# Normalising two chunks ahead in a spare scratch, a reordered end of the tile on ScalarE, and the products dealt over four steps

## The reference

```
mag = sqrt(a_re^2 + a_im^2); scale = min(mag, 0.999) / (mag + 1e-6)
a_re, a_im = a_re * scale, a_im * scale                  # "normalising"
for t in range(768):
    S = (a_re + i a_im)[t] * S + outer(k[t], v[t])        # complex state per head
    y[t] = q[t] @ real(S)
h = y @ w_in; e = exp(h - max(h)); solu = h * e / sum(e)
x = layernorm(solu) * g_ln @ w_out
noisy = x @ w_gate + softplus(x @ w_noise) * noise; top 2 experts, their softmax weights
out = sum over the token's 2 experts of weight * relu(x @ w1[e]) @ w2[e]
```

## Time and profile before

| | us |
|---|---|
| three runs | 1211.77, 1214.07, 1214.28 |
| median | 1214.07 |
| the profiled execution, its own time | 1212.83 |
| its span from first to last instruction | 1211.1 |
| PE busy, share of the span | 1041.4 (86%) |
| DVE busy | 872.8 (72%) |
| ACT busy | 621.1 (51%) |
| POOL busy | 449.7 (37%) |

### The profile page before, as it was taken

The page is one execution under the profiler, slowest core; times in us unless marked ns, Lnnn a source line. Parts: engine busy times, 40 slices in busy tenths (PEclk is TensorE's granted clock), DMA queues, the critical chain, the costliest instruction groups (busy, mean ns, idle before and its releaser), DMA issues.

```text
span 1211.1 us, 21883 instructions
## 1 busy us (share of the span) xinstructions
PE 1041.4 (86%) x7866; PEld 984.5 (81%) x7866; DVE 872.8 (72%) x1729; ACT 621.1 (51%) x967; POOL 449.7 (37%) x417
## 2 busy tenths in 40 slices
PE   0046988988998998899964999999999999999996
PEld 0035887877887887788864999999999999999996
DVE  6888779879969969945553777667676767776672
ACT  6432663764664664544532555555555555555551
POOL 4110241252352352243523244345434533543442
PEclk9977998998898898899986999999999999999998
DMA  9420220230230210211404666767676767676640
GB/s 231 174 76 27 54 86 27 67 86 27 66 87 27 64 37 27 58 42 53 125 14 156 227 233 226 253 234 256 202 267 235 253 227 244 228 230 235 209 162 1
DMA packets 85980, 167.51 MB, mean 138 GB/s; under 512 B 18566, under 2 KB 57696, under 8 KB 85872
## 3 DMA queue, kind: packets, MB, share of 16 engines
q1 hardware_dynamic: 72432, 137.71, 36.1%
q0 software_dynamic: 13440, 28.40, 6.4%
HBM read 148.83 MB, written 21.92 MB: 141 GB/s over the span
## 4 chain that ended last, share of the span: by engine, by line
PE 55%; issue 2%; ACT 1%; DVE 1%; DMA 1%; POOL 0%; POOLq 0%; DVEq 0%; ACTq 0%; SPq 0%
PE bank L1367 22%; PE bank L1547 21%; PE bank L1411 3%; PE bank L1358 3%; PE bank L1459 3%; PE bank L1433 1%; PE bank L1491 1%; PE bank L1471 0%; ACT z L859 0%; DMA xg<-xs,mine 0%; PE bank L1477 0%; PE bank L1387 0%; DMA tags<-tag,idx 0%; ACT x L856 0%; ACT x2t L867 0%
## 5 line engine op out<-in xcount | busy, mean ns | idle before, releaser
L899 ACT ACTIVATE hh<-bank 128x256 fp32r<-128x256 f32 x248 | 95.3, 384 | 256.6 <-PE bank L1367 256.6
L1367 PE MATMUL bank<-sxh,w1h 128*128 128x256 f32 x744 | 212.1, 285 | 2.1 <-DVE sxl L1317 2.1
L1367 PE MATMUL bank<-sxh,w1l 128*128 128x256 f32 x744 | 210.3, 283 | 0.0
L1367 PE MATMUL bank<-sxl,w1h 128*128 128x256 f32 x744 | 210.0, 282 | 0.0
L1336 DVE SCALAR_TENSOR_TENSOR hl<-bank,hh 128x256 fp32r<-128x256 f32 x248 | 104.8, 423 | 120.8 <-ACT hh L899 109.0
L672 POOL DMA_INDIRECT out<-yo,mine x62 | 77.9, 1256 | 277.8 <-DVE yo L1329 268.4
L1547 PE MATMUL bank<-w2h,hh 128*128 128x384 f32 x496 | 167.4, 337 | 0.0
L1547 PE MATMUL bank<-w2l,hh 128*128 128x384 f32 x496 | 166.8, 336 | 0.0
L1547 PE MATMUL bank<-w2h,hl 128*128 128x384 f32 x496 | 166.6, 336 | 0.0
L1367 PEld LDWEIGHTS bank<-sxh,w1h 128*128 128x128 f32 x744 | 140.8, 189 | 2.5 <-DVE sxl L1317 2.5
L1367 PEld LDWEIGHTS bank<-sxh,w1l 128*128 128x128 f32 x744 | 141.5, 190 | 0.0
(11 more groups left out here) (184 smaller groups left out, 2353.4 us busy)
## 6 DMA issues: line engine op xcount, KB each, us to landing
raw<-in_w SPq DMA_DIRECT2D x62, 1536.0 KB
ar<-in_a_re SPq DMA_DIRECT2D x6, 768.0 KB, 4.7
turn<-in_a_im SPq DMA_DIRECT2D x6, 768.0 KB, 7.0
qk<-in_q SPq DMA_DIRECT2D x48, 96.0 KB, 2.4
qk<-in_k SPq DMA_DIRECT2D x48, 96.0 KB, 2.5
out<-wide SPq DMA_DIRECT2D x9, 512.0 KB, 11.3
vt<-in_v SPq DMA_DIRECT2D x24, 192.0 KB, 2.6
xs<-x SPq DMA_DIRECT2D x24, 192.0 KB, 2.7
```

The source lines that it names most:

```text
L899: nc.scalar.activation(hh[:, f % NH, :], bank[:, f % 2, 0:CAP], ACT.Relu).then_inc(hh_done, 1)
L1367: ins = MM(dst, stationary[a_](cc), moving[b_](cc), start=(n_ == 0), stop=(n_ == len(terms) - 1))
```

## The change

1. A scratch `magnitude` is laid over the `xg` buffers, which only the experts use. From chunk 2 on (q of 4 and more) `squares`, `m2`, `logs`, `zsum`, `scale` and `norm` work in it instead of in `cums`. It holds one half q at a time.
2. These are done for chunk c+2 in steps b = 1, 2 and 3 of chunk c, where before they were done for chunk c+1 in steps b = 3, 0 and 1. `neg` and `products_start` move from step b = 1 to b = 0 (chunk 1's stay at b = 1 of chunk 0).
3. `PRODUCTS` deals the 63 product instructions as 12, 28, 17 and 6 over the four steps from chunk 1 on, where it was 0, 20, 33 and 10; in chunk 0 the shares stay. Within the step on DVE, `fill(6)` ahead of the state's addition goes, at most 10 products stand between `kp` and `xl`, and what is left follows `qp`.
4. The second `newton` of a chunk moves from the end of step b = 3 to behind `zl` in the next step b = 0.
5. The tile's end on ACT becomes `x2`, `x2t`, centred z, `xh`, square. The square goes to SBUF (`squared`), so that `hidden` on PE no longer waits for it. In step b = 3 the first `inverse` stands ahead of `x2t`.
6. `xg` is cleared at n = T instead of at the start.

```diff
+        magnitude = nc.alloc_sbuf_tensor_at("magnitude", [P, 2, 2 * NG, HALF * BI], F32, offset=xg_at)
...
+        def mag(q, s_):
+
+            return cum_part(q, s_) if q < 4 else magnitude[:, s_]
...
-        PRODUCTS = (0, 20, 53, 63)
+        PRODUCTS = ((0, 20, 53, 63), (12, 40, 57, 63))
... (POOL)
-                if b == 0 and prep and c > 0:
-                    m2(2 * c + 3)
+                if b == 1 and c + 2 < C:
+                    m2(2 * c + 4)
+                if b == 3 and c + 2 < C:
+                    zsum(2 * c + 5)
                 if has(m):
...
-                if b == 0 and prep and c > 0:
-                    zsum(2 * c + 2)
...
-                if b == 0 and prep and c > 0:
-                    zsum(2 * c + 3)
-                if b == 3 and c + 2 < C:
-                    m2(2 * c + 4)
+                if b == 1 and c + 2 < C:
+                    zsum(2 * c + 4)
+                if b == 2 and c + 2 < C:
+                    m2(2 * c + 5)
... (ACT)
-                wait(act, qp_done, 2 * B * (u - 1))
-                wait(act, kp_done, 2 * B * (u - 1))
+                if q >= 4:
+                    act.wait_ge(an_done, 3 * q)
...
-                ahead = b == 0 and prep and c > 0
+                ahead = c + 2 < C
+                starting = prep and b == (1 if c == 0 else 0)
...
-                if ahead:
-                    squares(2 * c + 3)
-                    logs(2 * c + 2)
-                if b == 1 and prep:
+                if starting:
                     neg(2 * c + 2)
                     neg(2 * c + 3)
+                if b == 1 and ahead:
+                    squares(2 * c + 4)
+                if b == 2 and ahead:
+                    scale(2 * c + 4)
+                if b == 3 and ahead:
+                    logs(2 * c + 5)
...
-                if ahead:
-                    logs(2 * c + 3)
+                if b == 1 and ahead:
+                    logs(2 * c + 4)
+                if b == 2 and ahead:
+                    squares(2 * c + 5)
...
+                if b == 3 and ahead:
+                    scale(2 * c + 5)
...
-                    nc.scalar.activation(bank[:, 4:6, :].rearrange("p b x -> p (b x)"), z[:], ACT.Square,
-                                         accum_out=mv[i % 2][:, 2:3]).then_inc(var_done, 1)
+                if b == 3 and prep:
+                    inverse(2 * c + 2)
...
+                if has(i):
+                    act.wait_ge(centred, i + 1)
+                    nc.scalar.activation(squared[:], z[:], ACT.Square, accum_out=mv[i % 2][:, 2:3]).then_inc(var_done, 1)
... (DVE)
+                if b == 0 and 0 < c < C:
+                    newton(2 * c + 1)
...
-                if b == 1 and prep:
+                if first_one:
                     norm(2 * c + 2)
                     norm(2 * c + 3)
+                if b == 0 and 0 < c < C - 1:
+                    products_start(c + 1)
+                if b == 2 and c + 2 < C:
+                    norm(2 * c + 4)
...
-                    fill(share - 20 - made[0] if b == 2 else share)
+                    fill((4, 10, 5, share)[b])
...
-                fill(6)
...
+                if b == 3 and c + 2 < C:
+                    norm(2 * c + 5)
+                fill(10)
...
-                    newton(2 * c + 3)
... (PE)
-                    wait(pe, var_done, i)
+                    wait(pe, solu_step, 4 * i)
                     hidden(0, 6 * NP)
```

## The result

The changed kernel takes 1195.1 us in the median of four runs (1193.6 to 1196.8), the kernel before 1212.9 beside it. The ratio is 0.9866, with a 95% interval of 0.9845 to 0.9888: faster by 1.3%, clear of the noise, and inside the range, but with less than half of the forecast gain. The time lies 1.1 us above the 1194 of the rival "DVE becomes the bound with POOL's sums in its way".

The account below looks back on a forecast made before the run. Outside the PE-bound experts, PE's waits in the steps and their clock cost were taken as the loss. Gains 278.3 - 252.0 + 92.0 - 81.5 - 1.5 + 2.5 = 37.8 us gave 1176 us, range 1162 to 1196.

Parts of the forecast that it names:

- DVE becomes the bound with POOL's sums in its way: Rival, chance 0.20: collisions cost about 13 us a chunk instead of 8.5, chunks take 88.5, total 1194 us.
- the base of each step: DVE's fixed work in every step, 9.6 us: 9.05 from step 21 plus 0.55 for the state's addition.
- chunk 4: Chunk without norm, square or log: 81.5 us forecast against 92.0 before.
- the forecast of 84.0: Time of each of chunks 1 to 3, summed from their four steps, against 92.8 on average before.
- step 13: Second step of chunk 3: 28 products on DVE's base, 1.1 us of waiting, 1.5 for POOL's sums; 22.0 us, before 26.2.
- step 14: Third step of chunk 3: products, carries, a norm and 0.8 us of collisions; 20.2 us, before 23.2.
- step 15: Last step of chunk 3: 20.4 us, gain 0.7; DVE's 19.9 include about 2 of collisions; reorder on ACT gives nothing.
- the waits for `zh`: DVE's `zl` waited 4.0 us for `zh` in step 13; forecast to vanish in step b = 1.
- the disputed term: DVE time lost per chunk to collisions with POOL's work: kept at about the old 8.5 us, bounds 5 and 18.7.
- step 12: First step of chunk 3: 21.4 us, gain 0.3; SP's DMAs hold `weigh` to 17.4, DVE 1.5 to 2.5 to spare.
- chunk 0: Pays for two norms and leftovers behind `qp`: loss of 1.5 us, bounds a gain of 1 and a loss of 4.
- Tail: Step 25: logits no longer wait behind centred z and square for `x2t`; 2.5 us saved.

Follow-up runs that it names:

- experiment 3: The kernel before the change, with POOL's m2 and zsum from chunk 2 on adding only 8 of 768 elements; 1207.5 us, ratio 0.9963.
- experiment 5: The changed kernel with the scale and first inverse of step b = 3 on ACT moved behind x2, x2t and centred z; 1191.1 us, ratio 0.9812.
- experiment 11: The kernel before with only the change's end of the tile on ACT, hidden not waiting for the square; 1208.4 us, ratio 0.9995.
- experiment 8: The changed kernel with SP's cum and md spreads of step b = 3 issued ahead of the next q and k; 1189.1 us, ratio 0.9840.

## Why less than half of the forecast gain came

**Right: the base of each step, and chunk 4.** DVE's work, product by product, and what hides behind PE gave 81.5 for chunk 4, measured 81.7. With the sums cut, chunks 1 to 3 take 82.3, 84.0 and 82.8; the forecast of 84.0 holds 4.3 us of collisions (1.5 in step 13, 0.8 in step 14, about 2 in step 15), of which the 1.5 were for sums. Step 14 came out at 20.4 (20.2 forecast), and the waits for `zh` went and that for the scale fell from 3.5 us to 0.5. In chunk 3 PE stood for no `x2` and no scores behind squares or logs.

**Wrong: the disputed term.** The step that failed is "I take about the old 8.5, since `m2` and `zsum` leave step 12 but meet chains in 13 and 14". The stretches grew to about 12 us in chunk 3, and the sum of the steps held only the 4.3 above: step 13 has 5.9, step 14 1.1 and step 15 4.3. In this chunk two sums fell on chain products of step 13, and the other two not in step 14 but in step 15, on a carry and the CAST ahead of the maximum. The sums' share rose from 2.5 to 6, and was on the path: cutting them gives 5.4 to 7.2 us a chunk, and 4.7 in chunk 0, where the forecast named no collision. In all 25 us between the two traces (28 between the medians), against 8 and 4 in the kernel before.

I had written that 10 of the 16 POOL instructions met a waiting DVE and that DVE would wait much less, and then kept the loss. The four sums stretch DVE by 1.5 us each on average, near the 1.9 of their length. Taken at their whole length of 1.82, the four would have been put at 7.3 us a chunk, near what the cut gave. The Trainium skill (SBUF — State Buffer, "Who interferes with whom") states such an exclusion for a whole instruction, and the sums here bear it out. Such an exclusion alone does not tell what lies on the path: the 60 decays, which stretch DVE too, cost 7 us in all. The prediction also counted only POOL's sums and decays; the mask of `at` stretches DVE as well (1.25 at 354.56, 1.06 at 398.37).

**The price of a stretch was counted once.** A sum that delays DVE by 1.7 us in front of `xl` or the maximum also makes a gap on PE, after which the clock is at its lower level. The granted clock of chunk 3 rises from 0.92 to 1.00 when the sums are cut. An estimate from these two: 89.9 us at a mean of 0.92 hold about 14 us at half the clock, which do what 7 us do at the full one. So the clock's part of the 7.1 us that the cut gave in chunk 3 can be anything up to all of it; how they divide between stretch and clock stays open. In the kernel before the clock was as low with the sums as without (0.93 both), and chunk 3 gained nothing (experiment 3).

**Step 15: 20.4 forecast, 23.4 measured.** 4.3 us of stretch lie ahead of the maximum (a carry 1.3 and the CAST 1.6 beside sums, `hot` 0.8 beside the mask, `picked` 0.6 beside a decay), and it is 4.3 us later than without the sums. "About 2 are collisions" was the mis-sized term. With the sums cut, the step takes 21.2 us. The order on ACT, which I had put at nothing, took none of this step (experiment 5 leaves it at 23.4) but 0.7 of the one behind it.

**Step 13: 22.0 forecast, 23.7 measured.** 5.9 us of stretch stand here, 3.1 of them beside the two sums, where the forecast had 1.5. With the sums cut, the step takes 20.1 us.

**Step 12: 21.4 forecast, 22.4 measured.** `weigh` came 17.15 us behind the cut (17.4 forecast), but with the DMAs earlier it came at 16.7 and the step stayed: DVE was nearly as late as SP, and the spare 1.5 to 2.5 us did not exist. The 1.0 us over the forecast lies behind `weigh`, where `xl` waited 1.2 us for `xh` (0.3 before). PE began the hidden layer 2.3 us behind the cut (325.99 and 323.71; 1.2 before), at the same mean clock of 0.83 in both kernels. With ACT's other order in step b = 3 the wait is 0.7 and the step 21.7.

**Chunk 0: a loss of 1.5 forecast, 4.2 measured.** Its bound was 4. The sums cost 4.7 us. The norms and leftovers cost nothing over the three steps together; step 3 alone is 2.9 us longer than before without the sums, and steps 1 and 2 make up for it.

**Tail: 2.5 forecast, 6.2 measured,** nearly all by the end of the tile (5.8 in experiment 11). The waiting of 3.4 us and the square were right, but the hidden layer of step 25 also starts 1.6 us earlier behind the cut (589.52 - 572.62 = 16.9, before 600.99 - 582.48 = 18.5), and with a gap of 0.55 us ahead of it in place of 1.91 it keeps the higher clock and takes 5.7 us instead of 7.3.

**Not foreseen: steps 20 and 21 lose 3.5 us.** The prediction had no term for them. SP has issued the `rc` DMAs 15.6 us behind the cut of step 19 in both kernels, but DVE is ready for `weigh` at 12.4 (15.3 before). So it waits 6.3 us instead of 1.8, and `weigh` begins at 18.6 (17.1 before). PE stands 4.3 us ahead of the hidden layer (0.1 before) and takes 8.5 us for it (5.7). With the DMAs earlier all of it goes (experiment 8).

**How far the rival was right.** "DVE becomes the bound with POOL's sums in its way" names the cause that the cut shows, and with 13 us of stretch and 88.5 us a chunk it is near the 12 and the mean of 89.6. That its time is met within 1.1 us is luck in part: chunks 1 to 3 are 3.3 us longer in all than it has them, chunk 0 is 1.2 and steps 20 to 23 are 3.5 longer, while chunk 4 is 2.3 and the tail 3.7 shorter.

## What to carry to other kernels

Before work is moved into the idle time of an engine, list what another engine does at that time that excludes it: idle time that hides such collisions is not free, and when it is filled a collision can come back at nearly its full length: the sixteen sums cost 1.75 us each of about 1.9, the sixty decays far less than their length. Of a loss that is hidden now, ask what it costs once the cover is gone, and forecast with that and not with its present value. When two engines exclude each other, give the work to the faster one: here DVE did the sums in half the time, and lost less than it had lost by waiting.

A queue's order is checked from both ends: what a DMA that moves forward gains, and who waits for the one that it is moved past.

## What the runs showed of the hardware

A small DVE instruction with one input in SBUF was held too: a CAST of 8 elements took 1.81 us beside a POOL sum (396.53) and 0.15 without (373.16). A `TENSOR_REDUCE` out of PSUM, at 400.14, kept its 1.21 us beside two of POOL's decays (399.33 and 400.13).

POOL's mask of `at`, which has one input, held DVE as well: 1.25 us for a product of 0.35 (354.56, beside the mask at 354.50).

Six of SP's SBUF-to-SBUF DMAs took at least 3.7 us to issue (335.67 in the changed kernel, 0.62 each) and at most 5.0 (498.26), so that eighteen of them hold the queue for 12.3 us (327.02 to 339.36).
